# Keeping the network's columns in the attention's row order, with the reversal moved to the copies of x2

## What is computed

```python
attn = softmax(where(same_bucket(q, k), q @ k.T / 8, -1e9))          # per batch and head
x = (attn @ v).transpose(0, 2, 1, 3).reshape(B, S, 512)

X = np.fft.fft(x, axis=1)                                            # over the 768 rows
X = np.fft.fft(X, axis=2)                                            # over the 512 features
u = x + np.real(X)
un = (u - mean(u)) / np.sqrt(var(u) + 1e-06)                         # over the features
x2 = u + np.maximum(un @ w_ch1, 0.0) @ w_ch2                         # w_ch1 512 x 2048, w_ch2 2048 x 512

gate = sigmoid(causal_conv5(x2))                                     # 5 taps along the rows, per feature
out = (gate * (x2 @ w_val)) @ w_out
```

## Time and profile before

| | |
|---|---|
| three runs of the kernel before | 672.08, 672.52 (median), 674.57 us |
| span of the profiled execution | 672.3 us |
| PE busy | 638.7 us, 95% of the span |
| DVE, ACT, POOL busy | 364.8, 307.5, 250.7 us |
| share of PE in the chain that ended last | 81% |
| L1432 (opening the accumulators) | 128 PE records, 64 of them in one block of 7.04 us |

### The profile page before, as it was taken

The page is one execution under the profiler, slowest core; times in us unless marked ns, Lnnn a source line. Parts: engine busy times, 40 slices in busy tenths (PEclk is TensorE's granted clock), DMA queues, the critical chain, the costliest instruction groups (busy, mean ns, idle before and its releaser), DMA issues.

```text
span 672.3 us, 11293 instructions
## 1 busy us (share of the span) xinstructions
PE 638.7 (95%) x3810; PEld 512.0 (76%) x3810; DVE 364.8 (54%) x599; ACT 307.5 (46%) x586; POOL 250.7 (37%) x202
## 2 busy tenths in 40 slices
PE   2899999999999999888999999999999999996998
PEld 1667576766666675888888888889888888885786
DVE  3878786968778785987211111116333333369720
ACT  2877776868686773355322222223222222251132
POOL 6543333334252341844333333326444444342130
PEclk9999999999999999989999999999999999998899
DMA  5822231324132000100222221520222221000102
GB/s 125 248 71 71 71 94 47 94 68 112 56 91 71 0 25 1 48 1 0 64 63 62 62 62 62 188 63 30 65 62 62 62 62 47 1 0 1 62 32 94
DMA packets 34262, 42.08 MB, mean 63 GB/s; under 512 B 3520, under 2 KB 22208, under 8 KB 34240
## 3 DMA queue, kind: packets, MB, share of 16 engines
q1 hardware_dynamic: 32512, 37.77, 19.6%
q0 software_dynamic: 1728, 4.02, 2.3%
HBM read 38.63 MB, written 3.15 MB: 62 GB/s over the span
## 4 chain that ended last, share of the span: by engine, by line
PE 81%; DVE 11%; issue 3%; POOL 2%; ACT 1%; DMA 1%; SPq 0%; DVEq 0%; POOLq 0%; ACTq 0%
PE banks L1457 20%; PE banks L1445 20%; PE banks L1260 10%; PE banks L1243 10%; PE banks L1307 6%; PE banks L1552 5%; DVE row_min L927 2%; PE banks L1199 2%; PE banks L1536 2%; DVE x_then_u_then_gate L1135 2%; PE banks L1380 2%; PE banks L1432 1%; DVE x_then_u_then_gate L1132 1%; DVE probT L342 1%; DVE k_b L920 1%
## 5 line engine op out<-in xcount | busy, mean ns | idle before, releaser
L1122 DVE SCALAR_TENSOR_TENSOR h_lo<-banks,h_hi 128x512 fp32r<-128x512 f32 x64 | 35.5, 558 | 180.8 <-ACT h_hi L825 180.8
L927 DVE TENSOR_REDUCE row_min<-banks 128x1 f32<-128x768 f32 x96 | 91.3, 956 | 44.9 <-PE banks L1243 44.4
L676 ACT ACTIVATE prob<-banks,row_min 128x768 f32<-128x768 f32 x96 | 87.0, 906 | 30.7 <-DVE row_min L927 30.7
L1445 PE MATMUL banks<-unT_hi,w_hi 128*128 128x512 f32 (+1 forms) x256 | 86.3, 337 | 0.0
L1445 PE MATMUL banks<-unT_hi,w_lo 128*128 128x512 f32 (+1 forms) x256 | 86.2, 337 | 0.0
L1445 PE MATMUL banks<-unT_lo,w_hi 128*128 128x512 f32 (+1 forms) x256 | 86.1, 336 | 0.0
L1307 PE MATMUL banks<-ident,prob 128*128 128x128 f32 x576 | 79.7, 274 | 2.5 <-DVE probT L342 1.5
L501 POOL TENSOR_TENSOR k_b<-k_raw,k_a 64x768 fp32r<-64x768 f32 x16 | 29.2, 1826 | 125.6 <-ACT k_a L659 125.6
L1307 PEld LDWEIGHTS banks<-ident,prob 128*128 128x128 f32 x576 | 67.3, 140 | 10.3 <-ACT probT L342 2.6
L563 POOL TENSOR_TENSOR w_lo<-w_stage,w_hi 128x512 fp32r<-128x512 f32 x32 | 43.6, 1363 | 82.9 <-ACT w_hi L741 82.9
L1260 PE MATMUL banks<-probT,v_in 128*64 128x384 f32 x384 | 72.3, 498 | 0.7 <-ACT outT L686 0.7
(11 more groups left out here) (148 smaller groups left out, 1223.5 us busy)
## 6 DMA issues: line engine op xcount, KB each, us to landing
w_stage<-in_moe_w_ch SPq DMA_DIRECT2D x64, 256.0 KB, 2.9
q_raw<-in_q SPq DMA_DIRECT2D x32, 192.0 KB, 3.3
k_raw<-in_k SPq DMA_DIRECT2D x32, 192.0 KB, 3.6
v_in<-in_v SPq DMA_DIRECT2D x16, 192.0 KB, 2.4
out<-y_out SPq DMA_DIRECT2D x12, 256.0 KB, 2.0
seq_tables_sb<-in_dft POOLq DMA_DIRECT2D x6, 386.0 KB, 3.5
wvo_stage<-in_moe_w_val SPq DMA_DIRECT2D x1, 1024.0 KB, 5.2
wvo_stage<-in_moe_w_out SPq DMA_DIRECT2D x1, 1024.0 KB, 7.9
```

The lines of the kernel that those rows point to most:

```text
L676: act.activation(prob[s % 2][:, :, :], s_tile(s), ACT.Exp, bias=row_min[:, s:s + 1], scale=-1.0, accum_out=row_sum[:, s:s + 1]).then_inc(e ...
L927: dve.tensor_reduce(row_min[:, s:s + 1], s_tile(s), AX.XY, ALU.min).then_inc(min_ready, 1)
L1122: dve.scalar_tensor_tensor(out=h_lo[:, slot, at:at + size], in0=h_bank[c], scalar=0.0, in1=h_hi[:, slot, at:at + size].bitcast(F32), op0=A ...
L1445: op = pe.matmul(h_bank[c], w_[:, slot, kb, :], x_[:, kb, at:at + size], start=(kb == 0 and m == 0), stop=(kb == KB - 1 and m == 2))
```

## The change

The columns of `un_hi`, `un_lo`, the hidden blocks and the accumulators stay in the order of the attention's rows. `natural` and `reverse` are gone. `unT_hi` and `unT_lo` make one piece of every tile. `open_acc` takes one plain transpose for each tile and feature block (`is_transpose=True`), six for each d. The columns come into natural order in `take_x2`: the first half is a copy as before; the second half takes row 384 in a copy of one column, 127 columns read backwards, and 256 columns written backwards. That is four copies for each feature block where there were three. The rest of the difference is counts of semaphores (6 and 12 become 8 and 16; 9 becomes 7).

```diff
-        reverse = sb("reverse", [P, P])
...
-            pool.memset(reverse[:, :], 0.0).then_inc(consts_ready, 1)
-            pool.wait_ge(consts_ready, 7)
-            pool.affine_select(out=reverse[:, :], in_=reverse[:, :], compare_op=ALU.not_equal, fill=1.0,
-                               base=1 - P, pattern=[[1, P]], channel_multiplier=1).then_inc(consts_ready, 1)
+            pool.wait_ge(consts_ready, 6)
...
-                for rows, cols in natural(t):
-                    act.copy(un_hi[b][:, :, cols], src[:, :, rows]).then_inc(unT_hi_done, 1)
+                act.copy(un_hi[b][:, :, t * P:(t + 1) * P], src).then_inc(unT_hi_done, 1)
...
-                    act.copy(half[:, 0:C0 - HALF], PS[:, d, HALF:C0]).then_inc(x2_by_act, 1)
-                    act.copy(half[:, C0 - HALF:HALF], acc(d, 1)).then_inc(x2_by_act, 1)
+                    act.copy(half[:, 0:1], PS[:, d, HALF:HALF + 1]).then_inc(x2_by_act, 1)
+                    act.copy(half[:, C1 + 1:HALF], PS[:, d, C0 - 1:HALF:-1]).then_inc(x2_by_act, 1)
+                    act.copy(half[:, C1:0:-1], acc(d, 1)).then_inc(x2_by_act, 1)
...
-                low, high = c * C0, (C0, S)[c]
-                first = c == 0 or d % 2 == 0
-                for t in range(T):
-                    for rows, cols in natural(t):
-                        if cols.step == -1:
...
-                        pe.matmul(acc(d, c)[:, left - low:right - low], X[:, b, t, d * P:(d + 1) * P],
-                                  mover[:, at:at + right - left], start=first, stop=False, skip_group_check=True)
+                tiles = (range(C0 // P), range(C0 // P, T))[c]
+                for t in tiles:
+                    at = t * P - c * C0
+                    pe.matmul(acc(d, c)[:, at:at + P], X[:, b, t, d * P:(d + 1) * P], ident[:, :], is_transpose=True,
+                              start=(t == tiles[0] and (c == 0 or d % 2 == 0)), stop=False, skip_group_check=True)
```

More of the change, by code:

```diff
@@ L383, in un_bank @@
             return [1, 2, 3, 2, 3, 2, 3, 2, 4, 5, 4, 5][n]
[L385 to L396, removed]
         LAG = 3
@@ L507, in split_qk @@
                     .then_inc(lo_done, 1)
-            pool.wait_ge(consts_ready, 9)
+            pool.wait_ge(consts_ready, 7)
             scale_q(0, 0)
@@ L1035, in unT_lo @@
                 b, t = tile_at(n)
-                pieces = natural(t)
-                dve.wait_ge(unT_hi_done, unT_pieces(n))
+                dve.wait_ge(unT_hi_done, n + 1)
                 src = PS[:, un_bank(n), :].rearrange("p (k m) -> p k m", k=KB)
-                for rows, cols in pieces:
-                    dve.tensor_tensor(un_lo[b][:, :, cols], src[:, :, rows], un_hi[b][:, :, cols].bitcast(F32),
-                                      ALU.subtract).then_inc(unT_lo_done, 1)
+                cols = slice(t * P, (t + 1) * P)
+                dve.tensor_tensor(un_lo[b][:, :, cols], src, un_hi[b][:, :, cols].bitcast(F32),
+                                  ALU.subtract).then_inc(unT_lo_done, 1)
             def cos_and_sin(step):
@@ L1145, in take_x2 @@
                     half = x2[b][:, 2 * d + 1, PAD:PAD + HALF]
-                    dve.tensor_copy(half[:, 0:C0 - HALF], PS[:, d, HALF:C0]).then_inc(x2_by_dve, 1)
-                    dve.tensor_copy(half[:, C0 - HALF:HALF], acc(d, 1)).then_inc(x2_by_dve, 1)
+                    dve.tensor_copy(half[:, 0:1], PS[:, d, HALF:HALF + 1]).then_inc(x2_by_dve, 1)
+                    dve.tensor_copy(half[:, C1 + 1:HALF], PS[:, d, C0 - 1:HALF:-1]).then_inc(x2_by_dve, 1)
+                    dve.tensor_copy(half[:, C1:0:-1], acc(d, 1)).then_inc(x2_by_dve, 1)
             dve.wait_ge(taps_spread, 2)
@@ L1153, in _ @@
             take_x2(0)
-            dve.wait_ge(x2_by_act, 6)
+            dve.wait_ge(x2_by_act, 8)
             dve.wait_ge(x2_lead, B + 1)
@@ L1325, in pair @@
                             p_times_v(i - 1, g, part)
-            pe.wait_ge(consts_ready, 9)
+            pe.wait_ge(consts_ready, 7)
             pe.wait_ge(w_ready, 2)
@@ L1351, in transpose_un @@
                 if before is not None:
-                    pe.wait_ge(unT_lo_done, unT_pieces(before))
+                    pe.wait_ge(unT_lo_done, before + 1)
                 for kb in range(KB):
@@ L1416, in open_acc @@
             def open_acc(b, d, c):
-                low, high = c * C0, (C0, S)[c]
-                first = c == 0 or d % 2 == 0
-                for t in range(T):
-                    for rows, cols in natural(t):
-                        if cols.step == -1:
[L1424 to L1431, removed]
-                        pe.matmul(acc(d, c)[:, left - low:right - low], X[:, b, t, d * P:(d + 1) * P],
-                                  mover[:, at:at + right - left], start=first, stop=False, skip_group_check=True)
-                        first = False
+                tiles = (range(C0 // P), range(C0 // P, T))[c]
[3 more added lines that the diff above has]
+                              start=(t == tiles[0] and (c == 0 or d % 2 == 0)), stop=False, skip_group_check=True)
             def ffn1(n, b, slot):
@@ L1500, in _ @@
             ffn1(FB, 1, 0)
-            pe.wait_ge(x2_by_act, 6)
-            pe.wait_ge(x2_by_dve, 6)
+            pe.wait_ge(x2_by_act, 8)
+            pe.wait_ge(x2_by_dve, 8)
             for d in range(KB):
@@ L1523, in values @@
                     if d == 1:
-                        pe.wait_ge(x2_by_act, 12)
+                        pe.wait_ge(x2_by_act, 16)
                     if d == 2:
-                        pe.wait_ge(x2_by_dve, 12)
+                        pe.wait_ge(x2_by_dve, 16)
                 elif d == 0:
```

22 lines of the change are left out of this document (11 added, 11 removed).

## The result

The changed kernel takes 667.06 us (median of 4 runs, 666.76 to 668.4) against 672.3 us of the kernel before on the same chip; the ratio is 0.9915 with a 95% interval of 0.9895 to 0.9935, so 0.85% less time. On another chip, later, it was 666.96 against 673.27 us, ratio 0.9909 (0.9894 to 0.9925). The profiled executions are 666.7 and 672.3 us long, 5.6 apart.

A forecast was written before the change was run, and what follows sets the result against it. The prediction took PE, busy 95% of 672.3 us, to bound the kernel where it sets the pace. Savings of 4.40, 1.15 and 0.30 us less 0.20 us of copies gave 666.65, so 666.9 us as median; range 665.7 to 669.9.

The forecast's parts named there:

- What bounds the kernel: Whole kernel: PE busy 95% of 672.3 us; taking work from PE pays where PE sets the pace, including both accumulator openings.
- Batch 1's opening: Opening of batch 1's accumulators at 456.58 us: 24 one-record transposes, 2.64 us, replace 64 records, 7.04 us; saved 4.40 us.
- What was hidden under it: After batch 1's opening: `ffn1(17)` and `ffn1(18)` would not wait on DVE or POOL, so 4.4 us pass through whole.
- Rival 2: Batch change: late `relu_lo(17)` or POOL split makes `ffn1(18)` wait, gain given back, up to 671.3 us; chance 0.06.
- Batch 0's opening and tile 3: Before `ffn1(1)`: fewer PE records until DVE's wait takes over, 1.15 us saved; tile 3 whole in both batches, 0.3 us.
- The copies: `take_x2(1)` after the network: two more copy instructions per engine cost +0.2 us, bounds 0.1 and 0.8; hidden between batches.
- The sum: Whole kernel: 672.3 - 4.40 - 1.15 - 0.30 + 0.20 = 666.65 us for the profiled execution, 666.9 as median.
- Rival 1: Batch 0's opening, 310 to 320 us: PE half busy, clock falls to 0.50; 669.0 us, chance 0.36.
- a sign of being wrong: Changed kernel's profile: granted clock at 0.50 anywhere from 313 to 325 us would show the prediction wrong.
- the 1.7 us for half pace in `ffn1(1)`: After batch 0's opening: low clock lasts 3.4 us with PE fully busy, half of it lost, 1.7 us.
- its lower case: Clock fall in batch 0's opening, but clock back before `ffn1(1)`: 667.4 us instead of 669.0.
- Rivals 3 and 4: Transposes into open accumulators two records each, 669.5 us, chance 0.07; backward access in `take_x2(1)` slower, 676 or more, chance 0.03.

The follow-up runs named there:

- the repeat: The changed kernel measured again, unaltered, on another chip: 666.96 us, ratio 0.9909 to the kernel before.
- 3: Changed kernel with `unT_hi` and `unT_lo` making tile 3 in two pieces again, 127 columns and one: 669.76 us, one run.
- experiment 4: Changed kernel with x2's second half copied forwards as before, three forward copies for each feature block: 668.37 us, one run.
- experiment 6: Changed kernel with the unused tile `reverse` reserved again, so that SBUF addresses lie as before: 667.31 us, one run.
- 7: Changed kernel with the first convolution tap as a scalar_tensor_tensor with a column of zeros instead of a tensor_scalar: 668.09 us, ratio 0.9926.
- 8: Changed kernel with 24 zero-matrix matmuls added in two PE waits after the network: 665.14 us, ratio 0.9885; measured again, 666.19 us, ratio 0.9897.
- 9: Changed kernel with batch 1's 24 opening transposes made twice, the second pass overwriting the first: 669.60 us, one run.
- 1: Changed kernel with u brought in by ordinary float32 products with ident instead of transposes: 669.96 us, ratio 0.9948 to the kernel before.
- 2: Kernel before, without the single-column products in the opening of the accumulators: 670.27 us against 672.76, ratio 0.9960.

## Why the prediction was right, step by step

**What bounds the kernel.** As read: the two places in which PE's opening stood in the chain gave 5.6 us between them, and no other place moved by more than 0.2 us for a reason of the change.

**Batch 1's opening.** -4.40 forecast, -4.42 in the trace. Its two parts hold by themselves: a transpose is one record of 0.109 us (48 in 5.24), a product two (48 in 5.36), and a single column costs a whole record (-1.68 for 16).

**What was hidden under it.** 0.15 us of margin were left at `ffn1(17)`, forecast as small; 0.75 at `ffn1(18)`, forecast 0.6. Rival 2 had the right queue, and the margin held in every profile.

**Batch 0's opening and tile 3.** -1.15 and -0.3 were forecast, together -1.45; measured are -1.21 for the stretch in batch 1's tiles, tile 3's piece included (forecast 1.30), and -0.12 in batch 0's (0.15): -1.33. The wait on DVE took over where I put it: `relu_lo`'s first chunk was done at 320.40, as forecast, and `ffn1(1)` followed at 320.54. One wait on the way was not in the forecast: the transposes of T + 5 wait for DVE's `unT_lo` of T + 3, done at 317.67, which frees the banks they write, and so start at 317.82 instead of 317.7.

**The copies.** +0.2 forecast, +0.13 measured: 0.065 for each single-column copy, none for backward access.

**The sum.** -5.65 forecast, -5.62 in the trace, -5.24 by the first pair of medians and -6.31 by the second. It was made against the span, 672.3, which happened to lie near the median of the runs. A span and a time are not the same measure, though: the changed kernel's profiled execution has a time of 668.4 for its span of 666.7. So what carries over is the difference, and that the level came out (666.9 forecast, 667.06 measured) is in part luck. So is it that the two spans are 5.6 apart: three differences that are not the change's, -0.73, +0.32 and +0.4, happened to cancel.

**Rival 1, the clock.** Half right. It did not come about in the first profiled execution of the changed kernel, but it is real, and the repeat's shows what I had named as a sign of being wrong: the clock at 0.50 between 313 and 325. Nine profiled executions have the single transposes between the groups (the changed kernel twice, experiments 3, 4, 6, 7, 8 twice, 9), and in four of them the clock fell between 310 and 320. In the three with products there (before, 1, 2) it never did, but three are too few to show that the products prevent it. The more so as the fall at 296 comes and goes too: of the nine, the four that had it fell again here once, the five without it three times, and of the three with products two had it.

The price was mis-sized: I had 2.1 us; the stretch to `ffn1(1)` is longer by 0.36 (experiment 6), 0.18 (9), 0.99 (the repeat) and about 0.7 (3, its piece taken off). The term that failed is the 1.7 us for half pace in `ffn1(1)`: the clock was back before it in three, and at 320.0 in the repeat, 0.05 us after its start. At the low clock a group of four transposes takes 0.85 us instead of 0.45, PE is busy for most of the stretch (5.50 of 6.70 us), and the clock is back by its end. So rival 1 costs about what I gave as its lower case, 0.5 us, and came about in four of nine executions.

The rule of the Trainium skill that was put beside it ("TensorE: Matmul & The Clock Gate", Part 4), that a transpose doesn't count as PE-busy the same way, is not borne out. From 310.45 to 320.5 the changed kernel's PE was busy for 6.07 of 10.05 us, in 44 records that are all transposes, and the clock stayed at 2.4 GHz; so it did in five of the nine profiles. In three of the four others it rose again when PE had done nothing but transposes since the fall.

**Rivals 3 and 4** are out, by the 48 records of the changed kernel and by experiment 4.

**What stays open.** Batch 1's loop takes 129.5 or 129.93 us. Neither the addresses (6) nor the length of the opening (9) nor the kind of operation (the repeat) decides it. It is 0.06% of the time.

## What to carry to other kernels

Count a matrix engine's small operations by records, not by columns: where a float32 product only moves data, a transpose is half the price, and a product of one column is as dear as one of 128. A permutation is cheapest where it costs no extra instruction; here backward access in a copy was free, and only the cut at a single column showed. Where PE's work goes out of a stretch in which it waits anyway, the gain ends at the next engine's due time, so subtract that and not the work; and look whether the thinner stretch still keeps the clock.

## What the runs showed that was not expected

- A fall of the clock in a stretch of short bursts cost less than one ahead of dense work: 0.2 to 1.0 us in four executions, against 1.3 to 2.6 us at the output stage. At 1.2 GHz the bursts are longer and PE is busy for more of the time, and the clock was back before the dense work began, or within 0.05 us of it (in the repeat: fall at 313.1, back at 320.0, `ffn1(1)` at 319.96). Whether the longer bursts are what brings it back was not tested.
- 24 matmuls of a zero matrix, in two waits of 1.8 and 4.6 us, held the clock at 2.4 GHz (15.25 us for 66 products instead of 16.58 to 17.82).
- A convolution tap whose third operand is a broadcast column of zeros waits for POOL's operation just as the plain one did (5.88 against 5.69 us).
- Two executions of one program differ by 0.43 us in a loop of 744 matmuls that has no waits and the clock up.
